# Keys and layer input turned by VectorE and two transfers through memory, in place of TensorE transposes

## The reference, cut to what matters

```
for t in range(S):
    cur = einsum('bhd,bhe->bhde', u[None] * kt, vt)
    y[:, :, t] = einsum('bhd,bhde->bhe', rt, state + cur)
    state = wt[..., None] * state + einsum('bhd,bhe->bhde', kt, vt)
x = y as (3072, 384)
x = knee(x @ w_in) @ w_out          # w_in 384x2048, knee: 0, (h+1)^2/4 or h
out = (silu(x @ w_gate) * (x @ w_val)) @ w_out2   # 384x1536
```

## Time and profile before

| | |
|---|---|
| median of three runs | 964.13 us (964.03 to 966.61) |
| the profiled execution's own time | 965.67 us |
| its span on the core | 963.9 us |
| TensorE busy | 944.6 us (98%) |
| VectorE, ScalarE, GpSimd busy | 520.7, 402.8, 162.6 us |
| TensorE clock granted | 1.0 of full speed |

### The profile page before, as it was taken

One profiled execution on the slowest core, in us unless ns is written; L12 is line 12 of the kernel. 1 busy time (PEld: TensorE's weight loads), 2 busy tenths in 40 slices (PEclk: granted clock), 3 DMA queues, 4 the chain that ended last, 5 costly groups with the idle time before them and its releaser, 6 DMA issues.

```text
span 963.9 us, 20679 instructions
## 1 busy us (share of the span) xinstructions
PE 944.6 (98%) x8470; PEld 927.3 (96%) x8470; DVE 520.7 (54%) x909; ACT 402.8 (42%) x845; POOL 162.6 (17%) x155
## 2 busy tenths in 40 slices
PE   6899999999999999999999999999999999999997
PEld 5799999999999999999999999999999999999997
DVE  8997767667676675764444433334343333434333
ACT  4686455455554555544764322222222222222222
POOL 5993210302103012020454200000000000000000
PEclk9999999999999999999999999999999999999999
DMA  9824222231322313201333110010101001010000
GB/s 293 260 79 155 69 83 92 60 97 58 95 86 66 98 52 101 74 2 45 106 98 107 42 49 1 1 50 1 49 0 49 0 0 49 0 49 0 25 1 27
DMA packets 23506, 61.87 MB, mean 64 GB/s; under 512 B 2688, under 2 KB 12032, under 8 KB 23424
## 3 DMA queue, kind: packets, MB, share of 16 engines
q1 hardware_dynamic: 23424, 60.72, 19.7%
HBM read 51.27 MB, written 9.44 MB: 63 GB/s over the span
## 4 chain that ended last, share of the span: by engine, by line
PE 94%; DVE 3%; issue 1%; DMA 1%; ACT 0%; POOL 0%; SPq 0%; DVEq 0%
PE bank L1254 50%; PE bank L1282 35%; PE bank L1337 2%; PE bank L1313 2%; PE bank L1332 2%; PE bank L1343 1%; PE bank L1302 1%; DMA r_k_v_by_token<-in_rkv_token 1%; PE bank L1324 1%; DVE suf L1000 1%; DVE gate L1104 0%; DVE glo L1097 0%; PE bank L1299 0%; DVE k_r_by_channel L1025 0%; DVE w_by_channel L1010 0%
## 5 line engine op out<-in xcount | busy, mean ns | idle before, releaser
L841 ACT ACTIVATE ghi<-gate 128x384 fp32r<-128x384 f32 x224 | 117.2, 523 | 185.1 <-DVE gate L1116 95.3
L1097 DVE TENSOR_TENSOR glo<-gate,ghi 128x384 fp32r<-128x384 f32 x224 | 134.2, 599 | 106.7 <-ACT ghi L841 104.4
L1114 DVE TENSOR_TENSOR gate<-bank,gate 128x384 f32<-128x384 f32 x96 | 53.5, 557 | 215.1 <-ACT gate L960 215.1
L1254 PE MATMUL bank<-xhi,w2gv_ahi 128*128 128x384 f32 x480 | 161.3, 336 | 0.0
L1254 PE MATMUL bank<-xlo,w2gv_ahi 128*128 128x384 f32 x480 | 161.3, 336 | 0.0
L1254 PE MATMUL bank<-xhi,w2gv_alo 128*128 128x384 f32 x480 | 161.3, 336 | 0.0
L960 ACT ACTIVATE gate<-bank 128x384 f32<-128x384 f32 x96 | 47.2, 492 | 227.7 <-PE bank L1254 227.7
L1282 PE MATMUL bank<-ghi,w1ohi 128*128 128x384 f32 x384 | 133.9, 349 | 1.5 <-DVE glo L1097 1.5
L1254 PE MATMUL bank<-xhi,w1ihi 128*128 128x384 f32 x384 | 129.2, 336 | 2.3 <-DVE gate L1104 1.4
L1254 PE MATMUL bank<-xhi,w1ilo 128*128 128x384 f32 x384 | 129.1, 336 | 0.0
L1282 PE MATMUL bank<-glo,w1ohi 128*128 128x384 f32 x384 | 129.1, 336 | 0.0
(11 more groups left out here) (98 smaller groups left out, 1559.6 us busy)
## 6 DMA issues: line engine op xcount, KB each, us to landing
r_k_v_by_token<-in_rkv_token SPq DMA_DIRECT2D x21, 672.0 KB, 5.6
k_r_by_channel<-in_kr_channel SPq DMA_DIRECT2D x24, 448.0 KB, 4.8
w_by_channel<-in_w_channel SPq DMA_DIRECT2D x24, 226.2 KB, 2.8
x_t<-ring SPq DMA_DIRECT2D x8, 576.0 KB, 3.0
x_raw<-x_t SPq DMA_DIRECT2D x8, 576.0 KB, 4.1
ring<-in_w_out SPq DMA_DIRECT2D x21, 192.0 KB, 2.4
out_t<-ring SPq DMA_DIRECT2D x7, 576.0 KB, 3.1
ring<-in_w_in SPq DMA_DIRECT2D x12, 192.0 KB, 5.1
```

What stands on the lines that cost most here:

```text
L841: e.activation(ghi[j % 2][:, :], gate[j % 2][:, :], ACT.Copy).then_inc(M["hi", ph], 1)
L1097: e.tensor_tensor(glo[j % 2][:, :], gate[j % 2][:, :], ghi[j % 2][:, :].bitcast(F32), ALU.subtract)\
L1114: e.tensor_tensor(q, hid[j % 2][:, 0:T], q, ALU.mult).then_inc(M["t", 2], 1)
L1254: m = e.matmul(out, w_of(a, k), x_of(b_, k), start=start and i == 0, stop=stop and i == total - 1)
```

## The change

From group 2 on (`MOVED = 2`), `KT` and `XT` are gone from TensorE's list. VectorE turns k and x in blocks of 32x32 (`turn_k`, `turn_x`), which leaves each block in the block row where it was. SyncE then writes the blocks to a buffer in device memory, waits for that write (`k_out`, `x_out`), and reads them back with four transfers of 32 rows each, which puts each block in its place (`move_k`, `move_x`). `ST` takes k from the new tile `k_moved`, and ScalarE and VectorE split `xhi` and `xlo` from `x_moved` in SBUF (`split_moved`). A window's x is asked for three slots after it was turned. There is one tile for the turned blocks of k, one of x, and two each for what comes back. The slots of the attention move to 2, 4, 5, 7, 8, 10; the last split stands in slot 13, where the last `XT` stood in slot 12. SyncE's loads for group g+1 now stand between the moves. k and r are loaded with 128 rows, the added 16 zero.

```diff
+MOVED = 2
+VISITS_MOVED = [[("AT", 0, 0), ("AT", 0, 1)],
+                [("Y", 0, 0), ("ST", 0, 0)],
+                [("AT", 1, 0), ("AT", 1, 1)],
+                [("Y", 1, 0), ("ST", 1, 0)],
+                [("AT", 2, 0), ("AT", 2, 1)],
+                [("Y", 2, 0), ("ST", 2, 0)]]
+FILLS_MOVED = [f for visit in VISITS_MOVED for f in visit]
+NF, NF_MOVED = len(FILLS), len(FILLS_MOVED)
+K_BLOCK_SLOTS = {1: 0, 3: 1, 6: 2}
+X_SPLIT_SLOTS = {7: 0, 10: 1, 13: 2}
...
+WIN_SLOTS = visits_at((2, 4, 5, 7, 8, 10), VISITS_MOVED, FILLS_MOVED)
+WIN_FIRST = visits_at((4, 6, 7, 9, 10, 12, 13), VISITS, FILLS)
...
-                e.dma_start(kr[:, w, :, :, :], kr_d[g, w]).then_inc(ld["kr", w], 16)
+                    wait(fill, fills_before(g - 1) + fill_no(g - 1, "Y", w) + 1)
+                rows = P if moved(g) else PR
+                e.dma_start(kr_rows[0:rows, w, :, :, :], kr_d[g, w][0:rows]).then_inc(ld["kr", w], 16)
...
+            def move_k(g, w):
+
+                n = moves(g, w)
+                wait(k_turned, n + 1)
+                if n >= 2:
+                    g2, w2 = divmod(g * NW + w - 2, NW)
+                    wait(fill, fills_before(g2) + fill_no(g2, "ST", w2) + 1)
+                e.dma_start(kb_d, k_blk[:, :, :]).then_inc(k_out, 16)
+                wait(k_out, 16 * (n + 1))
+                for t in range(NB):
+                    e.dma_start(k_moved[n % 2][t * BLK:(t + 1) * BLK, :, :],
+                                kb_d[:, t, :].rearrange("(b i) x -> i b x", b=NB)).then_inc(k_landed, 16)
+
+            def move_x(g, w):
+
+                n = moves(g, w)
+                wait(x_turned, n + 1)
+                if n >= 2:
+                    wait(xl_out, g * NW + w - 1)
+                e.dma_start(xb_d, x_blk[:, :, :]).then_inc(x_out, 16)
+                wait(x_out, 16 * (n + 1))
+                for c in range(NB):
+                    e.dma_start(x_moved[n % 2][c * BLK:(c + 1) * BLK, :, :],
+                                xb_d[:, c, :].rearrange("(b i) x -> i b x", b=NB)).then_inc(x_landed, 16)
...
+            def attention_of(g, loads):
+
+                def then_load(load, w):
+                    if loads:
+                        load(g + 1, w)
+
+                move_k(g, 0)
+                then_load(load_w, 0)
+                move_k(g, 1)
+                then_load(load_w, 1)
+                move_x(g, 0)
+                then_load(load_kr, 0)
+                then_load(load_tok, 0)
+                move_k(g, 2)
+                then_load(load_w, 2)
+                for w in (1, 2):
+                    move_x(g, w)
+                    then_load(load_kr, w)
+                    then_load(load_tok, w)
...
+            def split_moved(g, w, parity):
+
+                n = moves(g, w)
+                e.wait_ge(x_landed, MOVE * (n + 1))
+                e.activation(by_block(xhi[parity][:, :, cols(w)]), moved_x(n), ACT.Copy).then_inc(xh_out, 1)
...
                     e.tensor_tensor(xn[:, w, :], src[:, 0:DM], r_tok(w), ALU.add).then_inc(y_out, 1)
+                    if moved(g):
+                        turn_x(g, w)
...
+            def turn_k(g, w):
+
+                n = moves(g, w)
+                if n == 0:
+                    e.wait_ge(wlo, 2 * J1 - 1)
+                    e.wait_ge(wlo_d, 1)
+                else:
+                    e.wait_ge(k_landed, MOVE * n)
+                e.wait_ge(scaled, 2 * (g * NW + w) + 1)
+                e.transpose(k_blk.rearrange("q t (p j) -> q p t j", p=NPAIR),
+                            kr_rows[:, w, 0, :, :].rearrange("q p (t i) -> q p t i", t=NB)).then_inc(k_turned, 1)
+
+            def turn_x(g, w):
+
+                n = moves(g, w)
+                if n > 0:
+                    e.wait_ge(x_landed, MOVE * n)
+                e.wait_ge(y_out, g * NW + w + 1)
+                e.transpose(x_blk.rearrange("q c (k j) -> q k c j", k=KT),
+                            xn[:, w, :].rearrange("q (k c i) -> q k c i", k=KT, c=NB)).then_inc(x_turned, 1)
+
+            def split_moved(g, w, parity):
+
+                n = moves(g, w)
+                e.wait_ge(xh_out, g * NW + (w + 1))
+                e.wait_ge(x_landed, MOVE * (n + 1))
+                e.tensor_tensor(by_block(xlo[parity][:, :, cols(w)]), moved_x(n),
+                                by_block(xhi[parity][:, :, cols(w)].bitcast(F32)), ALU.subtract).then_inc(xl_out, 1)
...
+                    if j in K_BLOCK_SLOTS:
+                        turn_k(g + 1, K_BLOCK_SLOTS[j])
...
-                    e.wait_ge(kt_out, g * NW + (w + 1))
+                    n = moves(g, w)
+                    if moved(g):
+                        e.wait_ge(k_landed, MOVE * (n + 1))
+                    else:
+                        e.wait_ge(kt_out, g * NW + (w + 1))
                     e.wait_ge(ld["tok", w], (g + 1) * 16)
                     for h in range(2 * state_pairs(w, parity)):
                         p, r0 = h // 2, 64 * (h % 2)
                         for r in head_tiles(g):
                             rows = slice(r0 + r.start, r0 + r.stop)
-                            m = e.matmul(out[rows, p * D:(p + 1) * D], ktk[:, p * PR:(p + 1) * PR][:, rows],
+                            c0 = p * BLK
+                            k_rows = k_moved[n % 2][:, rows.start // BLK, c0:c0 + r.stop - r.start] if moved(g) else\
+                                ktk[:, p * PR:(p + 1) * PR][:, rows]
+                            m = e.matmul(out[rows, p * D:(p + 1) * D], k_rows,
                                          v_tok(w)[:, h * D:(h + 1) * D], start=True, stop=True)
                 elif kind == "Y":
                     e.wait_ge(ld["tok", w], (g + 1) * 16)
```

More of the change, by code:

```diff
@@ L80, with visits_at @@
 DIAG_SLOTS = {2: 0, 4: 1, 7: 2}
[L81 to L86, removed]
+def visits_at(slots, visits, order):
+    return {j: tuple(order.index(f) for f in visit) for j, visit in zip(slots, visits)}
+WIN_SLOTS = visits_at((2, 4, 5, 7, 8, 10), VISITS_MOVED, FILLS_MOVED)
+WIN_FIRST = visits_at((4, 6, 7, 9, 10, 12, 13), VISITS, FILLS)
 XT_FIRST = 13
@@ L116, in scan_slots, with moved, fills_before @@
     return SCAN_SLOTS_FIRST if first(g) else SCAN_SLOTS
+def moved(g):
+    return g >= MOVED
 def fills(g):
-    return FIRST_FILLS if first(g) else FILLS
+    return FIRST_FILLS if first(g) else FILLS_MOVED if moved(g) else FILLS
+def fills_before(g):
+    return min(g, MOVED) * NF + max(g - MOVED, 0) * NF_MOVED
 def fill_no(g, kind, w, n=0):
@@ L150, in build_program @@
         glo = [place(f"glo{i}", [P, T], F32R)[0] for i in range(2)]
-        ring, _ = place("ring", [P, KT + RING2, T], F32)
+        ring, ring_end = place("ring", [P, KT + RING2, T], F32)
         stage = ring[:, 0:KT, :]
@@ L177, in build_program @@
         suf, _ = place("suf", [PR, NW, WROW], F32)
-        kr, _ = place("k_r_by_channel", [PR, NW, 2, NPAIR, WIN], F32)
+        kr_rows, _ = place("k_r_by_channel", [P, NW, 2, NPAIR, WIN], F32)
+        kr = kr_rows[0:PR, :, :, :, :]
         last, _ = place("last_of_segment", [PR, WROW], F32)
@@ L187, in build_program @@
         xn, _ = place("x_by_token", [P, NW, DM], F32)
-        ring_b, _ = place("ring_b", [P, RING - KT - RING2, T], F32)
+        ring_b, o = place("ring_b", [P, RING - KT - RING2, T], F32)
+        k_blk, o = place("k_blocks", [P, NB, NPAIR * BLK], F32, o - (RING - KT - RING2) * T * 4)
+        x_blk, o = place("x_blocks", [P, NB, KT * BLK], F32, o)
+        k_moved = []
+        for i in range(2):
+            t, o = place(f"k_moved{i}", [P, NB, NPAIR * BLK], F32, o)
+            k_moved.append(t)
+        x_moved, o2 = [], ring_end - RING2 * T * 4
+        for i in range(2):
+            t, o2 = place(f"x_moved{i}", [P, NB, KT * BLK], F32, o2)
+            x_moved.append(t)
+        assert o <= at[0] and o2 <= ring_end
         dg, _ = place("diag", [P, NW, H], F32)
@@ L302, in y_two_ago, with by_block, moved_x, moves @@
             g2, w2 = divmod(g * NW + w - 2, NW)
-            return g2 * NF + fill_no(g2, "Y", w2) + 1
+            return fills_before(g2) + fill_no(g2, "Y", w2) + 1
         def st_before(g, w):
             g1, w1 = divmod(g * NW + w - 1, NW)
-            return g1 * NF + fill_no(g1, "ST", w1) + 1
+            return fills_before(g1) + fill_no(g1, "ST", w1) + 1
+        def by_block(a):
+            return a.rearrange("p k (b j) -> p k b j", b=NB)
+        def moved_x(n):
+            return x_moved[n % 2].rearrange("p b (k j) -> p k b j", k=KT)
+        def moves(g, w):
+            return (g - MOVED) * NW + w
         def cols(w):
@@ L624, in _ @@
                 load_w(2, w)
+            def attention_of(g, loads):
[15 more added lines that the diff above has]
+                    then_load(load_tok, w)
             def half(g, after_next):
-                if after_next:
+                if after_next and g == 0:
                     for w in range(NW):
[L630 to L634, removed]
+                        load_kr(2, w)
```

(12 more changed lines are left out.)

28 lines of the change are left out of this document (16 added, 12 removed).

## The result

| | time, us | ratio to before, 95% |
|---|---|---|
| before, in the same session | 964.66 (963.42 to 966.78, 20 runs) | |
| after | 968.1 (963.01 to 973.55, 20 runs) | 1.0034 (1.0019 to 1.0048) |
| forecast | 953.2 (951.0 to 962.0) | |

The change made the kernel slower by 0.34%, where I had it faster by 1.1%. The runs of the kernel after spread over 10.5 us, those of before over 3.4. The profiled execution of after took 963.01 us, the fastest of its runs, so it shows the loss at its smallest; a second profile further down took 973.81.

What follows compares the result with a forecast made beforehand. TensorE's list, played without holes, was taken as the bound. From the median 964.13 us, 11.9 us of saved transposes were subtracted and 1 us added for small overruns, giving 953.2 us, range 951 to 962.

Steps and rivals of the forecast that it cites:

- The saving: On TensorE's chain, dropping `KT` and `XT` saves 1.98 us per half, 11.9 us over six halves.
- The turns: On VectorE, six turns per half, 0.65 us for k and 0.5 for x, 3.5 us per half, in idle time.
- A move by itself: On SyncE's queue, write, wait and four overlapping reads take 6.0 us, bounds 5 and 12.
- the rival at 986 us: Moves that don't overlap: a 12 us move makes `ST` and the next group's `tile_in` wait; 986 us, chance 0.12.
- By this the moves are covered everywhere, with a margin of 1.3 to 2.4 us: Schedule of a half: every k and x lands before it is wanted; 1 us in all added for small overruns.
- the time of the second x, 39.5 us from slot 0: x of window 1: turned at 30.6, SyncE free at 33.5, landed at 39.5; called the tightest place.
- That price I had in the sum: SyncE's queue: next group's loads land at about 30.4; k of window 2 behind them is out at 31.3.
- 0.9 us for the first x: x of window 0: landed at 25.6, ScalarE asks at 26.5.
- 0.5 and 1.3 of margin: Around slot 10, second x: 0.5 us left ahead of `knee`, 1.3 between `lo` of tile 12 and `tile_out`.
- The rival "late second x": Moves take 1 us more, second x lands 3 us late, TensorE stops 1.2 us in five halves; 958.7, chance 0.18.
- The price of a stop: In the late second x rival, 1.2 us stops in five halves, less in the sixth, add 6.5 us.
- those margins: `ST` has 2.4 us left for k of window 0; the next group's first `tile_in` 1.5 us after the splits.

Runs made afterwards that it cites:

- a second profile: The changed kernel, unaltered, timed and profiled once more because its runs spread over 10 us: 973.81 us.
- the kernel with no moves: Changed kernel without the moves' transfers; VectorE turns straight into `k_moved` and `x_moved`, so values differ: 951.45 us, 0.9868 of before.
- the loads later: Changed kernel with the next group's loads of k, r and tokens issued behind the move of the second x: 953.26 us, 0.9884 of before.
- the longer scan: Kernel with the loads behind the second x, plus three more VectorE scans ahead of slot 10's scan in five halves: 979.46 us, 1.0170 of before.
- k ahead of the loads: Changed kernel with the move of k of window 2 ahead of the next group's first loads: 972.66 us, 1.0072 of before.
- the later scan: Changed kernel with VectorE's first scan in slot 11, not slot 10: 957.74 us, 0.9937 of before.

## Why the prediction was wrong

- **The saving** (1.98 us per half, 11.9): right. Measured 2.01, in the kernel with no moves.
- **The turns** (0.65 and 0.5): 0.70 and 0.58, and hidden, as forecast.
- **A move by itself** (6.0 us): right or a little high. The first k was turned at 105.26 and the turn that waits for its landing started at 110.74: 5.5 us. The four reads, issued mostly 0.47 us apart and landing after a median of 2.0 us each, overlap, and the rival at 986 us fell. The Trainium skill, page "DMA: Bandwidth & Descriptors", section "Rules for kernel authors", has transfers under 64 KB as mostly overhead. This trace agrees: 72 reads of 48 KB and 72 of 64 KB both have a median of 2.0 us, loads of 192 KB one of 2.5. But the overhead of four reads doesn't add up.
- **The failed step** is "By this the moves are covered everywhere, with a margin of 1.3 to 2.4 us", and in it the time of the second x, 39.5 us from slot 0. Slot 0 of the half shown starts at 96.39, so it landed at 43.3, 3.8 us late. Along SyncE's queue: the first x's write was issued 0.7 us late and took 3.25 us, not 2.3, and its four issues took 2.76, not 4 x 0.47 = 1.9; so the next group's loads went out 2.3 us late. The write of k behind them took 5.36 us. That price I had in the sum, even a little high, and k was out at 32.6, not 31.3. The write of the second x then took 3.05 us, not 2.3, and its last read 3.77, not 2.2. So the mis-sized terms are the two writes, the issues and the last read. (The margin was also thinner than that sentence has it: its own list leaves 0.9 us for the first x and 0.5 ahead of `knee`.) Both writes of x were issued 0.47 us behind a load of the decay (226 KB); in the sixth half, which has no such load, they took 1.9 and 2.0 us. I had added what the large loads cost, and taken for all else the price of a queue with little in it. Why the last read took 3.77 us stays open: with the loads later it took 1.9 at the same place, with loads issued right behind it too. With 3.8 us late, less 0.5 and 1.3 of margin, a stop of 2.0 us follows, and 0.4 more as TensorE asked that much sooner than I had it; 2.78 was measured.
- **The rival "late second x"** named this place, and that it decides in five halves. It had x 3 us late and the stop 1.2 us long: 958.7. Its mechanism is what happened, and its size was too small. The range from 951 to 962 left out stops of near 3 us, which both profiles of after have.
- **The price of a stop** was taken as its length. Behind most long ones TensorE ran at half clock for about 3 us, which adds 1.7 to 6.8 us. Of before no row shows this, as it has no stop.
- In both profiles of after `ST` never waited for k, the first `tile_in` of a group never for `xlo`: those margins held.

The kernel with the loads later is the best measured that has the whole change: 953.26 us, 1.2% faster than before. It lacks 1.8 us to the kernel with no moves at all.

## What to carry to other kernels

When a transfer on the way to a deadline shares a queue with bulk loads, price it with the bytes issued shortly ahead of it, not with its time in an empty queue, and put the bulk behind it, or several us ahead: here the place of 1.15 MB decided between 953 and 973 us, and 3.5 us or more behind those bytes a write mostly took its 2 us again. A margin of one or two us behind a chain of several such transfers is no margin. And where TensorE runs without holes, a stop of 3 us mostly cost more than 3 us here, by the clock behind it, so a change that saves little per stage must not risk one.

## What the runs showed of the hardware that I had not expected

Of the twelve stops of 2.75 to 3.65 us in the profiles of after (twice), the longer scan and k ahead of the loads, ten were followed by a stretch at a granted clock of 0.50, three to seven us long (in four it began 0.4 to 0.9 us before TensorE went on, in six 0.1 to 1.5 us after), and two were not: the first of the longer scan (2.75 us, ended at 148.74) and one of k ahead (2.90 us, ended at 214.40). The stops of 1.92 us and less, there and with the later scan, were followed by none. What parts the two from the ten stays open.

Issues vary: four reads of an x took 1.73 us to issue in one place (134.61) and 2.76 in another of the same half (119.83).
